# First-layer tiles in twos, with half-height fifth products side by side in the array

## Chip, cores and metric

The kernel runs on one core of one Trainium2 chip. The metric is the time on the device in microseconds, the median over runs. Profiles are single executions; times within one are counted from the start of its span.

## What is computed

```python
# attention part: a softmax over 7 taps per head, and a causal convolution with it
w = exp(weight_gen - max(weight_gen)) ; w = w / (sum(w) + 1e-9)      # (4, 4096, 8 heads, 7)
out[b, s, h, :] = sum_k w[b, s, h, k] * x_pad[b, s + k, h, :]         # 24 channels per head, 192 in all
# feed-forward part over 16384 tokens
h = x @ w_in                                                          # 192 -> 2048
g = where(h >= 1, h, where(h <= -1, 0, (h + 1)**2 / 4))
out = g @ w_out                                                       # 2048 -> 192
```

Both products are made from float32 values split into two parts, a high part in the type float32r and the rest (low), so that a product is high x high + low x high + high x low.

## The kernel before

**Tiling.** The 16384 tokens are taken in 32 groups of 512 tokens, and these in 16 pairs (b = 0, 1): the first and the last pair are written out, the others are a loop (over_pairs, L149). A group is four tokens on each of 128 partitions. The hidden width of 2048 is 16 tiles of 128 units (NT = 16).

**First layer.** The 192 input channels are 128 and a rest of 64. For each tile n, `hidden` (L570) makes five products of 128x128 weights by 128x512 columns into one PSUM bank (L581): main high x high, main low x high, main high x low, and two for the rest. The rest of 64 channels is stacked: the tile xt_rest holds the high parts on rows 0-63 and the low parts on rows 64-127, and in_rest_high and in_rest_low hold the same 64 rows of weights twice, on both halves. So the fourth product is high x high and high x low at once, and of the fifth (in_rest_low) only rows 0-63 (low x high) matter much.

**Gate.** ACT makes relu (L364) and its square (L370), DVE the gate in place in PSUM (L472), ACT the high part (L375, gate_high), DVE the low part (L478, gate_low). In a tile's step ACT does, in this order: relu of tile n, gate_high of tile n-1, in tile 2 the copies of the finished group's sums (take_cross, L390), square of tile n. DVE does gate_low of tile n-1, in tile 2 the sums (sum_outputs, L498), then the gate of tile n.

**Second layer.** `outputs` (L585, L601) makes, for tile n - 3 (LAG = 3), four times a product of 384 and one of 192 columns, into the four accumulator banks acc. In the last tile (15) of a group the 192-column product comes first. Tile 0 of a group waits, accumulator by accumulator, until DVE has summed the group before (out_summed).

**Banks.** Four PSUM banks (slot) are used in turn by tiles and transposes (uses, L167; slot_free, L200): each use waits until the use four back is finished, which for a tile is its gate_low and for a transpose the low part made by DVE (turned_rest, L482).

**Turns.** The next group's input is transposed on TensorE (turn, L557, L566) in two parts, behind the first layer of tiles 3 and 8 (TURN_AFTER); for the first two groups at other places (FIRST_TURNS_AFTER). ACT takes the high part (turned_top, L378, L382), DVE the low part (L487, L491). POOL makes the convolution that the turns read, a group or more ahead.

**Order on TensorE.** In each step: first layer of tile n, a turn if one is due, second layer of tile n - 3.

Of the kernel before, what the change touches and what calls it, by code (L numbers as in the profile page):

```python
# [13 lines left out]
F32 = mybir.dt.float32  # L14
F32R = mybir.dt.float32r
ALU = mybir.AluOpType
ACT = mybir.ActivationFunctionType
AX = mybir.AxisListType

P = 128  # L20
# [6 lines left out]
WARM_PRODUCTS, WARM_FROM = 10, 8  # L27
W_CHUNKS = 4
LAG = 3
TURN_AFTER = (3, 8)  # L30
FIRST_TURNS_AFTER = ((12, 14), (5, 10))
EVICT_AT = 2

SOFTMAX_AFTER = {3: (1,), 4: (2,), 6: (3, 4), 7: (5, 6)}
# [3 lines left out]
def build(nc, x, weight_gen, w_in, w_out, out):  # L38
# [7 lines left out]
    GT = TOK * P  # L46
# [3 lines left out]
    R = D - P  # L50
# [12 lines left out]
    with ExitStack() as ctx:  # L63
        def sb(name, shape, dt=F32):
            return ctx.enter_context(nc.sbuf_tensor(name, shape, dt))
# [19 lines left out]

        xt_high = [sb(f"xt_high{b}", [P, GT], F32R) for b in range(2)]
        xt_low = [sb(f"xt_low{b}", [P, GT], F32R) for b in range(2)]
        xt_rest = [sb(f"xt_rest{b}", [P, GT], F32R) for b in range(2)]

        in_main = sb("in_main", [P, FF])  # L90
# [4 lines left out]
        in_rest_high = sb("in_rest_high", [P, FF], F32R)  # L95
# [45 lines left out]
        def wait(eng, semaphore, pair, per_pair, offset):  # L141

            if isinstance(pair, int):
                if per_pair * pair + offset > 0:
                    eng.wait_ge(semaphore, per_pair * pair + offset)
            else:
                eng.wait_ge(semaphore, pair * per_pair + offset)
# [28 lines left out]
        def tile_slot(pair, b, n):  # L176
            return slot[(USES * b + uses(pair, b).index(("tile", n))) % SLOTS]

        def turn_slot(pair, b, part):

            if b == 0 and is_first(pair):
                return slot[2 + part]
            pair, b = before(pair, b)
            return slot[(USES * b + uses(pair, b).index(("turn", part))) % SLOTS]

        def before(pair, b):
            return (pair, 0) if b == 1 else (pair - 1, 1)
# [167 lines left out]
        @block.scalar  # L355
        def _(act):
            def exponent(pair, b):
                wait(act, softmax_step, pair, 2 * 5, 5 * b + 2)
                nc.scalar.activation(gen_exp[:], gen_shift[:], ACT.Exp).then_inc(exp_done, 1)

            def relu(pair, b, n):

                wait(act, hidden_done, pair, 2 * NT, NT * b + n + 1)
                nc.scalar.activation(half_relu[n % 2][:], tile_slot(pair, b, n)[:], ACT.Relu,  # L364
                                     scale=0.5, bias=0.5).then_inc(relu_done, 1)

            def squared(pair, b, n):
                wait(act, relu_done, pair, 2 * NT, NT * b + n + 1)
                wait(act, gate_done, pair, 2 * NT, NT * b + n - 1)
                nc.scalar.activation(square[n % 2][:], half_relu[n % 2][:], ACT.Square  # L370
                                     ).then_inc(square_done, 1)

            def gate_top(pair, b, n):
                wait(act, gate_done, pair, 2 * NT, NT * b + n + 1)
                nc.scalar.activation(gate_high[n % 4][:], tile_slot(pair, b, n)[:], ACT.Copy  # L375
                                     ).then_inc(gate_high_done, 1)

            def turned_top(pair, b, part):  # L378

                wait(act, turned, pair, 4, 2 * b + part + 1)  # L380
                dst = (xt_high, xt_rest)[part][b]
                nc.scalar.activation(dst[:], turn_slot(pair, b, part)[:], ACT.Copy  # L382
                                     ).then_inc(turned_high_done, 1)

            def take_cross(pair, b):

                for i in range(TOK):
                    wait(act, acc_done, pair, 2 * TOK, TOK * b + i + 1)
                    wait(act, out_summed, pair, 2 * TOK, TOK * (b - 1) + i + 1)
                    nc.scalar.activation(out_cross[:, i, :], acc[i][:, D:2 * D], ACT.Copy  # L390
                                         ).then_inc(cross_copied, 1)

            act.dma_start(gen_in[0][:].rearrange("p t k -> p (t k)"), w_runs[:, 0:TOK * HK]
                          ).then_inc(gen_loaded[0], 16)
            exponent(0, 0)

            for c in range(W_CHUNKS):
                cols = slice(c * CW, (c + 1) * CW)
                act.wait_ge(in_loaded[c], 48)
                for raw, high in ((in_main, in_main_high), (in_rest, in_rest_high)):  # L400
                    nc.scalar.activation(high[:, cols], raw[:, cols], ACT.Copy).then_inc(in_high_done, 1)

            def out_high(c):

                tiles = slice(c * CT, (c + 1) * CT)
                act.wait_ge(out_w_loaded[c], 16)
                nc.scalar.activation(out_parts[:, tiles, 0, :], out_raw[:, tiles, :], ACT.Copy
                                     ).then_inc(out_high_done, 1)

            out_high(0)  # L410
            out_high(1)
            turned_top(0, 0, 0)
            turned_top(0, 0, 1)
            exponent(0, 1)
            out_high(2)
            out_high(3)

            def body(pair):
                for b in range(2):
                    for n in range(NT):  # L420
                        relu(pair, b, n)
                        if n > 0:
                            gate_top(pair, b, n - 1)
                        elif not (b == 0 and is_first(pair)):
                            gate_top(*before(pair, b), NT - 1)
                        if n == EVICT_AT and not (b == 0 and is_first(pair)):
                            take_cross(*before(pair, b))
                        squared(pair, b, n)
                        if n == EXP_AFTER and not is_last(pair):
                            exponent(pair + 1, b)  # L430
                        if n in turn_after(pair, b):
                            turned_top(*after(pair, b), turn_after(pair, b).index(n))

            over_pairs(act, body)
            gate_top(PAIRS - 1, 1, NT - 1)
            take_cross(PAIRS - 1, 1)

        @block.vector
        def _(dve):
# [41 lines left out]

            def turned_rest(pair, b, part):  # L482

                wait(dve, turned_high_done, pair, 4, 2 * b + part + 1)
                src = turn_slot(pair, b, part)
                if part == 0:
                    nc.vector.tensor_tensor(xt_low[b][:], src[:], xt_high[b][:].bitcast(F32),  # L487
                                            ALU.subtract).then_inc(turned_low_done, 1)
                else:
                    low_rows = xt_rest[b][R:2 * R, :]  # L490
                    nc.vector.tensor_tensor(low_rows, src[R:2 * R, :], low_rows.bitcast(F32),  # L491
                                            ALU.subtract).then_inc(turned_low_done, 1)

            def sum_outputs(pair, b):
# [61 lines left out]
        def _(pe):  # L556
# [12 lines left out]

            def hidden(pair, b, n):  # L570

                slot_free(pe, pair, b, ("tile", n))
                if n == 0:
                    wait(pe, turned_low_done, pair, 4, 2 * b + 2)
                if b == 0 and is_first(pair) and n % CT == 0:
                    pe.wait_ge(in_low_done, 2 * (n // CT) + 2)
                units = slice(n * P, (n + 1) * P)
                products = ((in_main_high, xt_high), (in_main_low, xt_high), (in_main_high, xt_low),
                            (in_rest_high, xt_rest), (in_rest_low, xt_rest))
                for j, (w, xt) in enumerate(products):  # L580
                    ins = nc.tensor.matmul(tile_slot(pair, b, n)[:], w[:, units], xt[b][:],  # L581
                                           start=(j == 0), stop=(j == len(products) - 1))
                ins.then_inc(hidden_done, 1)

            def outputs(pair, b, n):  # L585

# [27 lines left out]
            def body(pair):  # L614
                for b in range(2):
                    for n in range(NT):
                        hidden(pair, b, n)
                        if n in turn_after(pair, b):
                            turn(*after(pair, b), turn_after(pair, b).index(n))
                        if n >= LAG:  # L620
                            outputs(pair, b, n - LAG)
                        elif not (b == 0 and is_first(pair)):
                            outputs(*before(pair, b), NT + n - LAG)

            over_pairs(pe, body)
            for n in range(NT - LAG, NT):
# [22 lines left out]
```

## Time and profile before

| | us |
|---|---|
| median of 3 runs | 1261.16 |
| lowest and highest run | 1260.84, 1261.38 |
| span of the profiled execution | 1259.3 |
| TensorE products busy in it | 1209.8 |
| ACT busy | 898.3 |
| DVE busy | 818.9 |
| POOL busy | 697.0 |

The span runs from the first to the last instruction of one execution. TensorE's products are pipelined: one starts before the end that is printed for the one before it, so the cost of a product in a string of them is the distance between two starts. PE is TensorE, PEld its weight loads, DVE VectorE, ACT ScalarE, POOL GpSimd. The granted clock of TensorE is 1.00 at 2.4 GHz.

### The profile page before, as it was taken

To read this page: it belongs to the slowest core of one execution; us is meant where nothing else is said; L and a number is where in the kernel's file an instruction comes from. 1 tells how busy PE (TensorE), PEld (TensorE's weight loads), DVE (VectorE), ACT (ScalarE), POOL (GpSimd) and SP (SyncE) were. 2 spreads that over 40 slices of the span, in tenths; PEclk is the share of its full clock that TensorE was granted. 3 is DMA by queue.
4 is the path that set the end of the run, shared out by engine and by line. 5 is a ranking of instruction groups with operands and counts; after the bars stand their busy time and mean duration, and the time that the engine had idled before them with its cause. 6 is when DMAs were issued, how large, how long until landed. Compare 5 with 4: busy or idle time off the path is not lost.

```text
span 1259.3 us, 21159 instructions
## 1 busy us (share of the span) xinstructions
PE 1209.8 (96%) x6932; PEld 1094.7 (87%) x6932; DVE 818.9 (65%) x1434; ACT 898.3 (71%) x1773; POOL 697.0 (55%) x450
## 2 busy tenths in 40 slices
PE   0699999999999999999999999999999999999998
PEld 0578999999999999999999999999999999999987
DVE  1886666666666666666666666666666666666565
ACT  0567777777777777777777777777777777777776
POOL 2496555775555775555776555676555676555500
PEclk9999999999999999999999999999999999999999
DMA  3311111001111101111101111101111100110000
GB/s 116 105 36 48 49 48 48 27 20 47 47 47 47 44 3 47 47 47 47 47 0 47 47 47 47 47 8 39 47 47 47 47 20 27 47 47 12 13 13 13
DMA packets 17426, 51.59 MB, mean 41 GB/s; under 512 B 1800, under 2 KB 8068, under 8 KB 17408
## 3 DMA queue, kind: packets, MB, share of 16 engines
q1 hardware_dynamic: 17264, 51.25, 11.9%
q8 instruction: 10, 0.16, 0.1%
q10 hardware_dynamic: 144, 0.11, 0.0%
q14 instruction: 8, 0.07, 0.0%
HBM read 38.77 MB, written 12.58 MB: 41 GB/s over the span
## 4 chain that ended last, share of the span: by engine, by line
PE 93%; SPq 3%; DVE 3%; DMA 1%; ACT 1%; issue 0%; DVEq 0%
PE slot L581 46%; PE acc L601 44%; PE slot L566 2%; SPq L240 1%; SPq L255 1%; DMA out_raw<-in_moe_w_out 1%; SPq L252 1%; DVE slot L472 1%; DVE gate_low L478 1%; DVE out_parts L515 0%; DVE in_main_low L508 0%; SPq L258 0%; DVE in_rest_low L508 0%; ACT gate_high L375 0%; SPq L223 0%
## 5 line engine op out<-in xcount | busy, mean ns | idle before, releaser
L601 PE MATMUL acc<-out_parts,gate_high 128*128 128x384 f32 x2048 | 616.4, 357 | 6.0 <-DVE gate_low L478 5.9
L478 DVE TENSOR_TENSOR gate_low<-slot,gate_high 128x512 fp32r<-128x512 f32 x512 | 353.7, 691 | 398.9 <-ACT gate_high L375 398.6
L601 PE MATMUL acc<-out_parts,gate_low 128*128 128x192 f32 x2048 | 513.7, 251 | 0.5 <-DVE gate_low L478 0.5
L364 ACT ACTIVATE half_relu<-slot 128x512 f32<-128x512 f32 x512 | 307.7, 601 | 288.5 <-PE slot L581 288.4
L601 PEld LDWEIGHTS acc<-out_parts,gate_high 128*128 128x128 f32 x2048 | 384.9, 188 | 27.1 <-DVE gate_low L478 8.4
L601 PEld LDWEIGHTS acc<-out_parts,gate_low 128*128 128x128 f32 x2048 | 390.3, 191 | 17.9 <-DVE gate_low L478 0.7
L472 DVE SCALAR_TENSOR_TENSOR slot<-slot,square 128x512 f32<-128x512 f32 x512 | 353.0, 690 | 3.9 <-ACT square L370 3.9
L370 ACT ACTIVATE square<-half_relu 128x512 f32<-128x512 f32 x512 | 325.2, 635 | 0.0
L375 ACT ACTIVATE gate_high<-slot 128x512 fp32r<-128x512 f32 x512 | 304.0, 594 | 25.6 <-DVE slot L472 25.4
L301 POOL TENSOR_TENSOR conv<-x_in,tap_w 128x768 f32<-128x768 f32 x31 | 47.8, 1542 | 482.3 <-DVE tap_w L462 468.4
L301 POOL TENSOR_TENSOR tap<-x_in,tap_w 128x768 f32<-128x768 f32 x186 | 289.6, 1564 | 0.0
L320 POOL TENSOR_TENSOR conv<-conv,tap 128x768 f32<-128x768 f32 x124 | 230.4, 1858 | 0.0
L581 PE MATMUL slot<-xt_high,in_main_high 128*128 128x512 f32 x512 | 211.7, 414 | 1.8 <-DVE xt_rest L491 1.5
L581 PE MATMUL slot<-xt_low,in_main_high 128*128 128x512 f32 x512 | 202.1, 395 | 0.0
L581 PE MATMUL slot<-xt_high,in_main_low 128*128 128x512 f32 x512 | 201.3, 393 | 0.0
L581 PE MATMUL slot<-xt_rest,in_rest_high 128*128 128x512 f32 x512 | 201.3, 393 | 0.0
L581 PE MATMUL slot<-xt_rest,in_rest_low 128*128 128x512 f32 x512 | 199.1, 389 | 0.0
L581 PEld LDWEIGHTS slot<-xt_rest,in_rest_low 128*128 128x128 f32 x512 | 96.2, 188 | 23.1
L581 PEld LDWEIGHTS slot<-xt_rest,in_rest_high 128*128 128x128 f32 x512 | 96.1, 188 | 22.3
L581 PEld LDWEIGHTS slot<-xt_low,in_main_high 128*128 128x128 f32 x512 | 96.3, 188 | 21.1
L581 PEld LDWEIGHTS slot<-xt_high,in_main_high 128*128 128x128 f32 x512 | 96.3, 188 | 2.6 <-DVE xt_rest L491 1.7
L581 PEld LDWEIGHTS slot<-xt_high,in_main_low 128*128 128x128 f32 x512 | 97.8, 191 | 0.1
(41 smaller groups left out, 493.4 us busy)
## 6 DMA issues: line engine op xcount, KB each, us to landing
x_in<-in_x SPq DMA_DIRECT2D x30, 960.0 KB
out<-out_sb SPq DMA_DIRECT2D x32, 384.0 KB, 2.6
gen_in<-in_weight_gen SPq DMA_DIRECT2D x31, 112.0 KB, 2.3
out_raw<-in_moe_w_out SPq DMA_DIRECT2D x4, 384.0 KB, 9.9
in_main<-in_moe_w_in SPq DMA_DIRECT2D x4, 256.0 KB, 4.7
in_rest<-in_moe_w_in SPq DMA_DIRECT2D x8, 128.0 KB, 7.6
x_in<-in_x SPq DMA_DIRECT2D x1, 768.0 KB
x_in<-in_x SPq DMA_DIRECT2D x4, 139.5 KB
```

The lines of the kernel that those rows point to most:

```text
L240: sp.dma_start(flat[lo + 1:lo + SEQ_PARTS, 0:before * D], x_runs[lo:lo + SEQ_PARTS - 1, (RUN - before) * D:RUN * D]).then_inc(x_loaded[b], 16)
L252: sp.dma_start(in_main[:, c * CW:(c + 1) * CW], w_in[0:P, c * CW:(c + 1) * CW]).then_inc(in_loaded[c], 16)
L301: ops.tensor_tensor(dst[:, :, 0:D].rearrange("p t (h c) -> p t h c", h=H), x_in[b][:, k:k + TOK, :].rearrange("p t (h c) -> p t h c", h=H) ...
L320: ops.tensor_tensor(to, conv[b][:, :, 0:D], tap[k % 3][:], ALU.add).then_inc(step_sem, 1)
L364: nc.scalar.activation(half_relu[n % 2][:], tile_slot(pair, b, n)[:], ACT.Relu, scale=0.5, bias=0.5).then_inc(relu_done, 1)
L370: nc.scalar.activation(square[n % 2][:], half_relu[n % 2][:], ACT.Square).then_inc(square_done, 1)
L375: nc.scalar.activation(gate_high[n % 4][:], tile_slot(pair, b, n)[:], ACT.Copy).then_inc(gate_high_done, 1)
L472: nc.vector.scalar_tensor_tensor(h[:], h[:], 1.0, square[n % 2][:], ALU.max, ALU.min).then_inc(gate_done, 1)
L478: nc.vector.tensor_tensor(gate_low[n % 4][:], tile_slot(pair, b, n)[:], gate_high[n % 4][:].bitcast(F32), ALU.subtract).then_inc(gate_low_ ...
L566: ins = nc.tensor.transpose(dst[:, i * P:(i + 1) * P], conv[b][:, i, part * P:(part + 1) * P], ident[:])
L581: ins = nc.tensor.matmul(tile_slot(pair, b, n)[:], w[:, units], xt[b][:], start=(j == 0), stop=(j == len(products) - 1))
L601: ins = nc.tensor.matmul(dst, stationary, moving, start=(n == 0 and j == 0), stop=(n == NT - 1 and j == 1))
```

## The change

Tiles are taken in twos, an even n and n + 1. `hidden` now makes four products for each tile. The fifth is moved into the new function `rest_lows`, which is called after the second layer in an even tile's step: it issues one product over rows 0-63 that ends the even tile's sum, and one over rows 64-127 that begins the odd tile's sum in its own PSUM bank. Then `hidden` of the odd tile adds four products to it, and the last one tells ACT that it is done. The high parts of the input's rest are needed on rows 64-127 too, so there is a tile xt_rest_top, and ACT copies the transposed rest in two halves of 64 rows instead of one of 128. The turns move to behind odd tiles.

```diff
-TURN_AFTER = (3, 8)
-FIRST_TURNS_AFTER = ((12, 14), (5, 10))
+TURN_AFTER = (3, 9)
+FIRST_TURNS_AFTER = ((11, 13), (5, 9))
...
+        xt_rest_top = [sb(f"xt_rest_top{b}", [P, GT], F32R) for b in range(2)]
...
-                dst = (xt_high, xt_rest)[part][b]
-                nc.scalar.activation(dst[:], turn_slot(pair, b, part)[:], ACT.Copy
-                                     ).then_inc(turned_high_done, 1)
+                src = turn_slot(pair, b, part)
+                if part == 0:
+                    nc.scalar.activation(xt_high[b][:], src[:], ACT.Copy).then_inc(turned_high_done, 1)
+                else:
+                    nc.scalar.activation(xt_rest_top[b][R:2 * R, :], src[R:2 * R, :], ACT.Copy
+                                         ).then_inc(turned_high_done, 1)
+                    nc.scalar.activation(xt_rest[b][0:R, :], src[0:R, :], ACT.Copy
+                                         ).then_inc(turned_high_done, 1)
...
-                wait(dve, turned_high_done, pair, 4, 2 * b + part + 1)
+                wait(dve, turned_high_done, pair, 6, 3 * b + 2 * part + 1)
...
-                    low_rows = xt_rest[b][R:2 * R, :]
-                    nc.vector.tensor_tensor(low_rows, src[R:2 * R, :], low_rows.bitcast(F32),
+                    nc.vector.tensor_tensor(xt_rest[b][R:2 * R, :], src[R:2 * R, :],
+                                            xt_rest_top[b][R:2 * R, :].bitcast(F32),
                                             ALU.subtract).then_inc(turned_low_done, 1)
...
-                slot_free(pe, pair, b, ("tile", n))
+                if n % 2 == 0:
+                    slot_free(pe, pair, b, ("tile", n))
...
-                            (in_rest_high, xt_rest), (in_rest_low, xt_rest))
+                            (in_rest_high, xt_rest))
                 for j, (w, xt) in enumerate(products):
+                    first, last = (j == 0, False) if n % 2 == 0 else (False, j == len(products) - 1)
                     ins = nc.tensor.matmul(tile_slot(pair, b, n)[:], w[:, units], xt[b][:],
-                                           start=(j == 0), stop=(j == len(products) - 1))
-                ins.then_inc(hidden_done, 1)
+                                           start=first, stop=last)
+                if n % 2:
+                    ins.then_inc(hidden_done, 1)
+
+            def rest_lows(pair, b, n):
+
+                slot_free(pe, pair, b, ("tile", n + 1))
+                if n == 0:
+                    wait(pe, turned_high_done, pair, 6, 3 * b + 3)
+                nc.tensor.matmul(tile_slot(pair, b, n)[:], in_rest_low[0:R, n * P:(n + 1) * P],
+                                 xt_rest[b][0:R, :], start=False, stop=True).then_inc(hidden_done, 1)
+                nc.tensor.matmul(tile_slot(pair, b, n + 1)[:],
+                                 in_rest_low[R:2 * R, (n + 1) * P:(n + 2) * P],
+                                 xt_rest_top[b][R:2 * R, :], start=True, stop=False)
...
                             outputs(*before(pair, b), NT + n - LAG)
+                        if n % 2 == 0:
+                            rest_lows(pair, b, n)
```

## Rows read from the trace of the kernel before

**Rows 1.** The page, part 1: busy time, share of the span, instructions.
```profile
PE 1209.8 (96%) x6932; PEld 1094.7 (87%) x6932; DVE 818.9 (65%) x1434; ACT 898.3 (71%) x1773; POOL 697.0 (55%) x450
```
**Rows 2.** The page, part 4: the chain that ended last, by line.
```profile
PE slot L581 46%; PE acc L601 44%; PE slot L566 2%; SPq L240 1%; SPq L255 1%; DMA out_raw<-in_moe_w_out 1%; SPq L252 1%; DVE slot L472 1%; DVE gate_low L478 1%; DVE out_parts L515 0%; DVE in_main_low L508 0%; SPq L258 0%; DVE in_rest_low L508 0%; ACT gate_high L375 0%; SPq L223 0%
```
**Rows 3.** Stretches, one of a pair of groups: window, its us, busy us, clock.
```profile
671.00:746.00 75.00, 75.00 (x433) 68.03 (x433) 49.41 (x88) 55.47 (x111) 44.25 (x28) 1.00 0.12 40
```
**Rows 4.** Timeline of TensorE: start, duration, line, out<-in; two tiles.
```profile
640.61 0.41 PE L581 MATMUL slot<-xt_high,in_main_high 128*128 128x512 f32 x1
...
641.55 0.39 PE L581 MATMUL slot<-xt_rest,in_rest_low 128*128 128x512 f32 x1
641.78 0.33 PE L601 MATMUL acc<-out_parts,gate_high 128*128 128x384 f32 x1
...
642.81 0.25 PE L601 MATMUL acc<-out_parts,gate_low 128*128 128x192 f32 x1
642.89 0.41 PE L581 MATMUL slot<-xt_high,in_main_high 128*128 128x512 f32 x1
643.15 0.39 PE L581 MATMUL slot<-xt_high,in_main_low 128*128 128x512 f32 x1
...
645.19 0.41 PE L581 MATMUL slot<-xt_high,in_main_high 128*128 128x512 f32 x1
```
**Rows 5.** Timeline of TensorE's weight loads, same place.
```profile
642.81 0.19 PEld L581 LDWEIGHTS slot<-xt_high,in_main_high 128*128 128x128 f32 x1
642.92 0.19 PEld L581 LDWEIGHTS slot<-xt_high,in_main_low 128*128 128x128 f32 x1
```
**Rows 6.** Timeline of TensorE, first group: products behind an idle stretch.
```profile
67.20 0.47 PE L581 MATMUL slot<-xt_high,in_main_high 128*128 128x512 f32 x1 [0.34 <-DVE in_rest_low L508]
67.50 0.40 PE L581 MATMUL slot<-xt_high,in_main_low 128*128 128x512 f32 x1
```
**Rows 7.** Timeline of TensorE, start of a group: tiles 2 and 3.
```profile
620.29 0.25 PE L601 MATMUL acc<-out_parts,gate_low 128*128 128x192 f32 x1
...
622.61 0.60 PE L566 MATMUL slot<-ident,conv 128*128 128x128 f32 x4
622.97 0.42 PE L601 MATMUL acc<-out_parts,gate_high 128*128 128x384 f32 x1
```
**Rows 8.** Timeline of ACT: tile 2 of that group, and a later tile.
```profile
620.49 0.60 ACT L364 ACTIVATE half_relu<-slot 128x512 f32<-128x512 f32 x1 [0.69 <-PE slot L581]
620.98 0.59 ACT L375 ACTIVATE gate_high<-slot 128x512 fp32r<-128x512 f32 x1
621.46 1.01 ACT L390 ACTIVATE out_cross<-acc 128x192 f32<-128x192 f32 x4
...
641.98 0.60 ACT L364 ACTIVATE half_relu<-slot 128x512 f32<-128x512 f32 x1 [0.68 <-PE slot L581]
```
**Rows 9.** Timeline of DVE: tile 2 of that group.
```profile
621.61 0.69 DVE L478 TENSOR_TENSOR gate_low<-slot,gate_high 128x512 fp32r<-128x512 f32 x1 [0.99 <-ACT gate_high L375]
622.22 1.14 DVE L498 TENSOR_TENSOR out_sb<-acc,out_cross 128x192 f32<-128x192 f32 x4
```
**Rows 10.** Waits of the whole span: who waited for whom, us, times, longest.
```profile
PE acc L601 <- DVE gate_low L478: 6.4, 4, 3.7
```
**Rows 11.** Groups by line, 600 to 1000 us: the turned rest, the main part.
```profile
L491 DVE TENSOR_TENSOR xt_rest<-slot,xt_rest 64x512 fp32r<-64x512 f32 x11 | 7.6, 695 | 0.3
L487 DVE TENSOR_TENSOR xt_low<-slot,xt_high 128x512 fp32r<-128x512 f32 x10 | 6.8, 680 | 0.0
L382 ACT ACTIVATE xt_rest<-slot 128x512 fp32r<-128x512 f32 x10 | 6.0, 600 | 0.0
```
**Rows 12.** Timeline at the end: the last tile's second layer.
```profile
1254.36 0.36 PE L601 MATMUL acc<-out_parts,gate_low 128*128 128x192 f32 x1 [0.47 <-DVE gate_low L478]
```

## Prediction

> **What bounds the kernel now.** I read the page's busy times first: TensorE's products fill 1209.8 us of a span of 1259.3 us [rows 1]. The chain that ended last says the same by line: the first layer's products (L581) are 46% of the span, the second layer's (L601) 44% [rows 2]. The stretches settle it: from 671 to 746 us, which is one pair of groups, TensorE is busy 75.00 of 75.00 us at a granted clock of 1.00 [rows 3]. So the steady part is a string of matmuls, and the only price that counts is the distance from one start to the next. The durations printed (0.39 us and so on) overlap, so I never sum them.
>
> From the timeline of TensorE [rows 4]: a tile starts its first layer at 640.61 and the next at 642.89, 2.28 us; two tiles take 4.58 us. The fifth product starts at 641.55 and the second layer at 641.78, so that product costs 0.23 us. Two tiles' fifth products are 0.46 us: all that this change can touch on TensorE. A 192-column product costs 0.08 (642.81 to 642.89), the second layer of a tile 1.11, and four first-layer products 0.94.
>
> **The pair of half-height products.** There are 32 groups of 16 tiles, so 256 pairs. Call c what the two 64-row products cost together, from the first one's start to the start of the next tile's first product. The pairs give 256 x (c - 0.46) us. The trace has no product on 64 rows, so c has to be bounded.
> - Lower end: both stream at once and nothing is lost: one product, 0.23.
> - The second one needs its own weight load. Loads stand 0.11 us apart where they are closest (642.81 and 642.92) [rows 5], and a product starts 0.08 to 0.17 after its load. That puts the second product some 0.09 to 0.17 behind the first: c = 0.32 to 0.40.
> - No overlap at all: 0.46. The number of loads does not fall (26 in a pair, before and after).
> - If TensorE must empty itself on going from 128 rows to 64 and again on going back: a 192-column product ends, as modelled, 0.25 us after its start against 0.08 to the next start, and a 512-column one 0.39 against 0.23 [rows 4], so each crossing adds about 0.16: c = 0.23 + 0.32 = 0.55. A start from empty adds more: the tile at 67.20, which follows an idle stretch, has 0.30 to its second product, where 0.26 is usual [rows 6]. With that and the staggered second load c reaches about 0.8.
>
> I take c = 0.46. It is the middle of 0.23 and 0.68, and the nearest row in kind is the fifth product itself. It stands for a second product 0.17 behind the first and 0.06 lost at the borders, and equally for two products that don't overlap.
>
> The row for a change of kind speaks mildly for a cheap border: four transposes between first and second layer take 0.36 us (622.61 to 622.97), 0.09 each, hardly more than products of that width would, so there is no large gap at that change of mode [rows 7]. The Trainium skill speaks against the edit here: "TensorEngine Tiling (Array Packing)", section Key Properties, says that a change of tiling mode, as against a change of tile, makes TensorE drain. No row of this trace shows such a change; with that rule the time would be that of the second rival below.
>
> **What the new order does to the end of a group.** This is the part a busy share hides. Before, an even tile's first layer ended ahead of the second layer of three tiles back; now its last product comes behind it. Look at tile 2 of a group, where ACT also fetches the finished group's sums (L390). The second layer of the old group's tile 15 starts at 620.29 (known by its 192-column product coming first), and tile 2's relu on ACT at 620.49 [rows 7, 8]. ACT is in order: behind that relu stand gate_high of tile 1 (620.98) and then the four copies of the sums (from 621.46). DVE then does gate_low of tile 1 at 621.61 and the sums (L498) from 622.22, 1.73 us after the relu [rows 8, 9]. The first sum is done about 0.35 + 0.05 later, 2.13 after the relu (622.62), and the new group's first second-layer product, which overwrites that accumulator, starts at 622.97 [rows 7]. So the present slack is 0.35 us.
>
> Now tile 2's last product starts only after the 1.16 us of tile 15's second layer; call that start r. The relu comes 0.39 + 0.04 behind (as 641.55 to 641.98 does), so the first sum is ready at r + 0.43 + 2.13 = r + 2.56. TensorE is there at r + c + 0.94 + 0.36 (tile 3's four products, the transposes) = r + 1.30 + c. It waits 1.25 - c us: 1.02 at c = 0.23, 0.79 at 0.46. Everything on TensorE queues behind it. It happens in groups 1 to 31: 31 x (1.25 - c). The other sums follow each other faster (about 0.26) than TensorE asks for them (0.29), so only the first one counts.
>
> **Other places.** Today TensorE waits for gate_low 4 times, 6.4 us in all, at the two ends of the run [rows 10].
> - The slots: behind a transpose a tile takes the slot of three tiles back. Tile 6 needs gate_low of tile 3, which stands on ACT behind tile 4's relu: 0.43 + 0.49 + 0.63 + 0.69 + 0.05 = 2.29 us after tile 4's half-height product, and TensorE arrives c + 0.94 + 1.11 = 2.05 + c after it. Nothing for c of 0.24 or more; the same for tile 12. The wait of the pair for the odd tile's slot sits behind a second layer that needs the same gate_low or an earlier stall: nothing.
> - One more copy on ACT per group (0.60 us, 64 rows costing what 128 do by L491 against L487, 695 and 680 ns) [rows 11]: it lies behind tile 9's square, and ACT idles 0.68 us before each relu there, some 2 us over the next tiles [rows 8]. DVE's subtraction waits only for the first half. Nothing. In the opening it delays the exponent and the weights' split by up to 0.5 us, hidden or not.
> - The turns at 9 instead of 8 and the first ones at 11 and 13: the convolution they read is done long before. Nothing.
> - The last tile: its chain through ACT now starts behind tile 14's. TensorE waited before tile 15's second layer until 1254.36, 0.47 us [rows 12]; some 0.5 to 1 us more. I take 1.
>
> **Sum.** The span is 1259.3 us and the median of the runs 1261.16, 1.9 us more; I add the change to the median. Time = 1261.2 + 256 (c - 0.46) + 31 (1.25 - c) + 1 = 1183.2 + 225 c. At c = 0.46: 1286.7. Even where the pair is perfect the wait at the group's start takes back 32 us of 59. The kernel gains only if c is under 0.35.
>
> **Rivals.**
> - It gains: the two products really run side by side, c = 0.23 to 0.33. For it: loads are taken ahead of running products in this trace [rows 5], and there is no visible gap at the transposes. Against it: the loads are spaced 0.11, and both borders must be free. It decides at c = 0.35. 1235 to 1257, at best 1234.9. The skill's "TensorE: Matmul & The Clock Gate", Part 3, says tiles at different rows start some 4 ns apart; that would be this rival's best end, and no run so far shows it.
> - TensorE empties at both borders: c = 0.55 to 0.82, the time 1307 to 1368, at 0.68 1336. For it: two crossings per pair are 512 chances to lose 0.16. Against it: the transposes.
> - The pair costs as forecast, but the wait at the group's start is not there (ACT or DVE has more room than I read): 1261.2 + 256 x 0 + 1 = 1262, no change. Against it: ACT's order is fixed in the program, and its rows carry the 1.73 us.
> - That the edit does not do what it says, two half-height products one after the other, is inside the forecast (c = 0.46).
>
> **Chances.** Forecast, c from 0.34 to 0.54 (1260 to 1305, likeliest 1286.7): 0.37. Gain: 0.28. Emptying: 0.28. No wait at the start of a group: 0.07. The range leaves out the best tip of the first rival and the upper half of the second: 1237 to 1337. A difference under 0.2% (2.5 us) could not be told from none; for that strip around c = 0.35 and the third rival I give 0.09. Faster 0.28, slower 0.63.
>
> **What would show it.** In the changed profile: (1) the distance from the first half-height product to the next tile's first one is c; (2) the distance between the starts of the two tells overlap from stagger; (3) a distance over 0.09 from the last 192-column product to the first half-height one is a border loss; (4) TensorE idles 0.8 us before the first second-layer product of each group behind DVE L498, 31 times; (5) the granted clock stays 1.00; (6) a pair of tiles takes 4.12 us + c. I am wrong if c is under 0.34 or over 0.54, or if (4) is missing or larger than 1.3 us.

## The result, and the profile after

| | us |
|---|---|
| before, median | 1261.0 |
| after, median of 4 runs | 1334.47 (1332.88 to 1335.25) |
| ratio after to before | 1.0581 (95% interval 1.0566 to 1.0596) |
| span of the profiled execution, after | 1331.1 |

The change costs 73.5 us. The direction was forecast and the size was not: 1286.7 had been predicted, 26 us over the kernel before. The time lies just inside the upper end of the range, in the second rival's field.

The page of the kernel after, part 1 (busy time, share, instructions) and one line of part 4 (the chain that ended last, by line):

```profile
PE 1261.5 (95%) x6932; PEld 1050.6 (79%) x6932; DVE 820.2 (62%) x1434; ACT 922.1 (69%) x1805; POOL 696.4 (52%) x450
...
PE acc L621 43%; PE slot L589 36%; PE slot L599 8%; ACT gate_high L376 2%; PE slot L572 1%; DVE out_sb L504 1%; SPq L241 1%; SPq L256 1%; DMA out_raw<-in_moe_w_out 1%; SPq L253 1%; DVE gate_low L484 1%; ACTq L148 0%; DVE slot L478 0%; DVEq L148 0%; SPq L259 0%
```

In the kernel after, L589 is the first layer, L599 and L601 are the two half-height products, L621 is the second layer and L572 the transposes; on ACT, L365 is the relu, L376 gate_high and L396 the copies of the sums; on DVE, L484 is gate_low and L504 the sums.

TensorE still has most of the chain that ended last, with as many products as before ([rows 1], x6932) and 52 us more of busy time. Two things are new: the half-height products have 8% of the chain by themselves (L599), and gate_high on ACT (L376, 2%) and the sums on DVE (L504, 1%) stand in it; before, gate_high had under 1% and the sums nothing [rows 2].

A stretch of TensorE's timeline in the kernel after (start, duration, line, output<-inputs), the end of an even tile's step and the odd tile's first layer. It answers to [rows 4]:

```profile
644.46 0.25 PE L621 MATMUL acc<-out_parts,gate_low 128*128 128x192 f32 x1
644.63 0.50 PE L599 MATMUL slot<-xt_rest,in_rest_low 64*128 64x512 f32 x1
644.64 0.50 PE L601 MATMUL slot<-xt_rest_top,in_rest_low 64*128 64x512 f32 x1
645.07 0.50 PE L589 MATMUL slot<-xt_high,in_main_high 128*128 128x512 f32 x1
645.40 0.40 PE L589 MATMUL slot<-xt_high,in_main_low 128*128 128x512 f32 x1
...
649.37 0.50 PE L599 MATMUL slot<-xt_rest,in_rest_low 64*128 64x512 f32 x1
```

The two half-height products start together (644.63, 644.64). So the change does what it says. But the first one starts 0.17 us after the 192-column product (0.08 is usual), the next 128-row product 0.43 after them (0.23 is usual), and the one behind that 0.33 after (0.23). A border is a place where the string goes from products on 128 rows to products on 64, or back. At the two borders 0.09 + 0.20 + 0.10 = 0.39 us are lost, against 0.23 saved. From pair to pair it is 4.74 us, where it was 4.58 [rows 4].

The weight loads in the same place show what goes with it. A bracket is idle time ahead of a load, and "issue" means that no semaphore held it:

```profile
644.63 0.18 PEld L599 LDWEIGHTS slot<-xt_rest,in_rest_low 64*128 64x128 f32 x1 [0.16 <-issue]
644.64 0.18 PEld L601 LDWEIGHTS slot<-xt_rest_top,in_rest_low 64*128 64x128 f32 x1
645.06 0.19 PEld L589 LDWEIGHTS slot<-xt_high,in_main_high 128*128 128x128 f32 x1 [0.24 <-issue]
645.17 0.19 PEld L589 LDWEIGHTS slot<-xt_high,in_main_low 128*128 128x128 f32 x1
```

In the rest of the string a load is taken ahead, while the product before it runs (642.92 for the product at 643.15, rows 4 and 5 of before). At a border the load starts with its own product: it was not taken ahead. The two half-height loads start together, on different rows.

The other new cost is at the start of a group, where the timeline of TensorE, ACT and DVE together (kernel after) answers to [rows 7] to [rows 9]:

```profile
693.87 0.50 PE L599 MATMUL slot<-xt_rest,in_rest_low 64*128 64x512 f32 x1
...
694.40 0.60 ACT L365 ACTIVATE half_relu<-slot 128x512 f32<-128x512 f32 x1 [1.20 <-PE slot L599]
...
694.90 0.60 ACT L376 ACTIVATE gate_high<-slot 128x512 fp32r<-128x512 f32 x1
...
695.33 0.60 PE L572 MATMUL slot<-ident,conv 128*128 128x128 f32 x4
695.38 1.01 ACT L396 ACTIVATE out_cross<-acc 128x192 f32<-128x192 f32 x4
...
696.13 1.14 DVE L504 TENSOR_TENSOR out_sb<-acc,out_cross 128x192 f32<-128x192 f32 x4
...
696.54 0.44 PE L621 MATMUL acc<-out_parts,gate_high 128*128 128x384 f32 x1 [0.60 <-DVE out_sb L504]
```

From tile 2's relu (694.40) to the first sum on DVE (696.13) it is 1.73 us, as in the kernel before. TensorE has issued its transposes at 695.33; they take 0.36, so it could have gone on at 695.69 and goes on at 696.54: 0.85 us. The waits of the whole span (who waited for whom, us, times, longest) have it 31 times, in every group but the first; their microseconds are counted from the modelled end of a product, so they are shorter than the 0.85 by starts:

```profile
PEld acc L621 <- DVE out_sb L504: 23.2, 28, 0.8
PE acc L621 <- DVE out_sb L504: 19.5, 31, 1.1
DVE xt_rest L496 <- ACT xt_rest L388: 14.7, 32, 0.5
```

The last line is a small miss of mine and shows no cost on the path: DVE's subtraction waits for both copies of the turned rest, not for the first alone, and idles 0.46 us a group.

### The profile page after: what moved, and what is told of

Its sections match the earlier page's. It is cut to its first block, busy times and chain, and to the rows that moved or that the text cites. A ratio compares the mean times of both kernels' runs of the same rounds, so it can differ in the third digit from the quotient of the medians.

```text
span 1331.1 us, 21222 instructions
## 1 busy us (share of the span) xinstructions
PE 1261.5 (95%) x6932; PEld 1050.6 (79%) x6932; DVE 820.2 (62%) x1434; ACT 922.1 (69%) x1805; POOL 696.4 (52%) x450
## 4 chain that ended last, share of the span: by engine, by line
PE 89%; SPq 3%; DVE 3%; issue 2%; ACT 2%; DMA 1%; ACTq 0%; DVEq 0%
PE acc L621 43%; PE slot L589 36%; PE slot L599 8%; ACT gate_high L376 2%; PE slot L572 1%; DVE out_sb L504 1%; SPq L241 1%; SPq L256 1%; DMA out_raw<-in_moe_w_out 1%; SPq L253 1%; DVE gate_low L484 1%; ACTq L148 0%; DVE slot L478 0%; DVEq L148 0%; SPq L259 0%
## 5 line engine op out<-in xcount | busy, mean ns | idle before, releaser
L621 PE MATMUL acc<-out_parts,gate_high 128*128 128x384 f32 x2048 | 617.8, 357 | 23.8 <-DVE out_sb L504 19.5
L484 DVE TENSOR_TENSOR gate_low<-slot,gate_high 128x512 fp32r<-128x512 f32 x512 | 353.7, 691 | 455.7 <-ACT gate_high L376 455.7
L621 PE MATMUL acc<-out_parts,gate_low 128*128 128x192 f32 x2048 | 513.7, 251 | 0.6 <-DVE gate_low L484 0.6
L365 ACT ACTIVATE half_relu<-slot 128x512 f32<-128x512 f32 x512 | 308.1, 602 | 259.4 <-PE slot L599 259.4
L621 PEld LDWEIGHTS acc<-out_parts,gate_high 128*128 128x128 f32 x2048 | 384.9, 188 | 53.2 <-DVE out_sb L504 23.2
L621 PEld LDWEIGHTS acc<-out_parts,gate_low 128*128 128x128 f32 x2048 | 390.4, 191 | 20.0 <-DVE gate_low L484 0.8
L376 ACT ACTIVATE gate_high<-slot 128x512 fp32r<-128x512 f32 x512 | 304.8, 595 | 102.5 <-DVE slot L478 102.5
L589 PE MATMUL slot<-xt_high,in_main_high 128*128 128x512 f32 x512 | 235.9, 461 | 2.6 <-DVE xt_rest L496 2.2
L589 PE MATMUL slot<-xt_high,in_main_low 128*128 128x512 f32 x512 | 203.7, 398 | 0.0
L589 PE MATMUL slot<-xt_low,in_main_high 128*128 128x512 f32 x512 | 202.6, 396 | 0.0
L589 PE MATMUL slot<-xt_rest,in_rest_high 128*128 128x512 f32 x512 | 201.9, 394 | 0.0
L589 PEld LDWEIGHTS slot<-xt_high,in_main_high 128*128 128x128 f32 x512 | 96.0, 187 | 66.0 <-issue 63.5
L601 PE MATMUL slot<-xt_rest_top,in_rest_low 64*128 64x512 f32 x256 | 127.6, 498 | 0.0
L599 PE MATMUL slot<-xt_rest,in_rest_low 64*128 64x512 f32 x256 | 126.7, 495 | 0.0
L589 PEld LDWEIGHTS slot<-xt_rest,in_rest_high 128*128 128x128 f32 x512 | 96.5, 189 | 23.9
L589 PEld LDWEIGHTS slot<-xt_low,in_main_high 128*128 128x128 f32 x512 | 96.6, 189 | 23.0
L589 PEld LDWEIGHTS slot<-xt_high,in_main_low 128*128 128x128 f32 x512 | 97.6, 191 | 0.1
```

The lines of the kernel that those rows point to most:

```text
L484: nc.vector.tensor_tensor(gate_low[n % 4][:], tile_slot(pair, b, n)[:], gate_high[n % 4][:].bitcast(F32), ALU.subtract).then_inc(gate_low_ ...
L599: nc.tensor.matmul(tile_slot(pair, b, n)[:], in_rest_low[0:R, n * P:(n + 1) * P], xt_rest[b][0:R, :], start=False, stop=True).then_inc(hid ...
L601: nc.tensor.matmul(tile_slot(pair, b, n + 1)[:], in_rest_low[R:2 * R, (n + 1) * P:(n + 2) * P], xt_rest_top[b][R:2 * R, :], start=True, st ...
L621: ins = nc.tensor.matmul(dst, stationary, moving, start=(n == 0 and j == 0), stop=(n == NT - 1 and j == 1))
```

## The experiments

Theory A: the loss is two separate prices, the borders between 128-row and 64-row products (some 0.18 us per pair beyond what the overlap saves) and the wait at the start of 31 groups. Rivals: the new order alone, or half-height products slow in themselves, or never side by side.

**The new order without half-height products.** Both products of `rest_lows` over all rows:

```diff
-                nc.tensor.matmul(tile_slot(pair, b, n)[:], in_rest_low[0:R, n * P:(n + 1) * P],
-                                 xt_rest[b][0:R, :], start=False, stop=True).then_inc(hidden_done, 1)
+                nc.tensor.matmul(tile_slot(pair, b, n)[:], in_rest_low[:, n * P:(n + 1) * P],
+                                 xt_rest[b][:], start=False, stop=True).then_inc(hidden_done, 1)
...
-                                 in_rest_low[R:2 * R, (n + 1) * P:(n + 2) * P],
-                                 xt_rest_top[b][R:2 * R, :], start=True, stop=False)
+                                 in_rest_low[:, (n + 1) * P:(n + 2) * P],
+                                 xt_rest[b][:], start=True, stop=False)
```

> The changed kernel's order, but both products of rest_lows run over all 128 rows, as the fifth product did before. Same sums as in the kernel before, no 64-row product anywhere. Theory A (two parts: the borders between 128-row and 64-row products cost 0.175 us per pair net of the overlap, 45 us in all, and the wait at the start of a group costs about 0.85 us, 31 times, 26 us): the borders go, the wait stays or grows by 0.05, so 1261 + 31 x 0.9 + 1, about 1290. Rival B (the loss is made by the new order alone, in waits on ACT and DVE, and the half-height products cost no more than one product): 1334 or more, since this kernel has one product more per pair.

Measured: 1290.67 us, ratio 1.0231 (1.0214 to 1.0248). Its two fifth products run one after the other, so TensorE has the time of one product more per pair, and it is 43.8 us faster than the changed kernel. The same place in this kernel, TensorE's timeline, and its waits:

```profile
645.85 0.25 PE L621 MATMUL acc<-out_parts,gate_low 128*128 128x192 f32 x1
645.94 0.41 PE L599 MATMUL slot<-xt_rest,in_rest_low 128*128 128x512 f32 x1
646.20 0.39 PE L601 MATMUL slot<-xt_rest,in_rest_low 128*128 128x512 f32 x1
646.42 0.40 PE L589 MATMUL slot<-xt_high,in_main_high 128*128 128x512 f32 x1
646.66 0.40 PE L589 MATMUL slot<-xt_high,in_main_low 128*128 128x512 f32 x1
```
```profile
PE acc L621 <- DVE out_sb L504: 18.9, 31, 1.1
```

No border, and the 31 waits are all there. The rival that the order alone makes the loss is out. The start of a group here, TensorE, ACT and DVE together:

```profile
673.87 0.39 PE L599 MATMUL slot<-xt_rest,in_rest_low 128*128 128x512 f32 x1
...
674.30 0.60 ACT L365 ACTIVATE half_relu<-slot 128x512 f32<-128x512 f32 x1 [1.02 <-PE slot L599]
...
675.26 0.60 PE L572 MATMUL slot<-ident,conv 128*128 128x128 f32 x4
676.03 1.14 DVE L504 TENSOR_TENSOR out_sb<-acc,out_cross 128x192 f32<-128x192 f32 x4
...
676.43 0.44 PE L621 MATMUL acc<-out_parts,gate_high 128*128 128x384 f32 x1 [0.57 <-DVE out_sb L504]
```

The relu comes 0.43 behind the even tile's fifth product, and TensorE waits from 675.62 (675.26 + 0.36) to 676.43: 0.81 us.

**The sums fetched first.** The changed kernel with ACT's copies and DVE's sums moved to the front of tile 2's step:

```diff
+                        if n == EVICT_AT and not (b == 0 and is_first(pair)):
+                            take_cross(*before(pair, b))
                         relu(pair, b, n)
                         if n > 0:
                             gate_top(pair, b, n - 1)
                         elif not (b == 0 and is_first(pair)):
                             gate_top(*before(pair, b), NT - 1)
-                        if n == EVICT_AT and not (b == 0 and is_first(pair)):
-                            take_cross(*before(pair, b))
...
+                        if n == EVICT_AT and not (b == 0 and is_first(pair)):
+                            sum_outputs(*before(pair, b))
                         if n > 0:
                             gate_rest(pair, b, n - 1)
```

> The changed kernel, with ACT's four copies of the finished group's sums put ahead of tile 2's relu, and DVE's sums ahead of gate_low of tile 1. Theory A: the first sum is ready before the pair of tile 2 is over, the 31 waits behind L504 vanish, about 26 us less than the changed kernel: 1308. Rival B (the wait only moves: the pair of tile 4 then waits for gate_low of tile 2): over 1325, and a new wait of about 0.8 us a little later in each group.

Measured: 1306.39 us, ratio 1.0356 (1.0339 to 1.0373). 28.1 us less than the changed kernel, 0.91 per group, and no wait of TensorE behind L504 is left in the trace. The wait did not move elsewhere; that rival, over 1325, is out.

**Both edits.**

> Both edits at once: the changed kernel's order with products over 128 rows, and the sums fetched ahead of tile 2's relu. If the borders and the wait at the group's start are all there is, this is back at the kernel before: 1261 to 1263. A rest of over 5 us would be a third cost of the new order.

Measured: 1259.28 us, ratio 0.9988 (0.9978 to 0.9998). There is no third cost. The four kernels make a square: the borders cost 43.8 us with the wait and 47.1 without it (0.17 and 0.18 per pair), the wait 28.1 us with the borders and 31.4 without (0.91 and 1.01 per group). The 1.01 is not all wait. By the traces a steady pair takes 4.58 us in the kernel with the new order alone (643.89 to 648.47) and 4.56 in this one (644.08 to 648.64), and 0.02 in each of 8 pairs is 0.16 us of a group.

**The pair of products ahead of the second layer.** The changed kernel with the call of `rest_lows` moved up by one step:

```diff
+                        if n % 2 == 0:
+                            rest_lows(pair, b, n)
                         if n >= LAG:
                             outputs(pair, b, n - LAG)
                         elif not (b == 0 and is_first(pair)):
                             outputs(*before(pair, b), NT + n - LAG)
-                        if n % 2 == 0:
-                            rest_lows(pair, b, n)
```

> The changed kernel, with rest_lows called ahead of the second layer instead of behind it, so a pair of half-height products stands between a 512-column product and a 384-column one. Theory A: tile 2's relu comes 1.1 us earlier against TensorE, so the wait at the group's start vanishes, the borders stay: about 1308, and a pair of tiles takes 4.75 us as in the changed kernel. Rival B (what is lost at a border depends on the neighbours, the short 192-column product in front hides part of it): over 1320.

Measured: 1311.05 us, ratio 1.0393 (1.0376 to 1.041), under the 1320 from which the border would have depended on its neighbours. Also in this way the wait at the group's start is gone and the borders stay, in other company: a 512-column product in front, the second layer behind. Two lines of its waits, and the border in its timeline:

```profile
PEld slot L599 <- DVE gate_low L484: 55.6, 128, 2.2
...
PE slot L599 <- DVE gate_low L484: 7.0, 29, 1.7
```
```profile
643.80 0.39 PE L589 MATMUL slot<-xt_rest,in_rest_high 128*128 128x512 f32 x1
644.12 0.50 PE L599 MATMUL slot<-xt_rest,in_rest_low 64*128 64x512 f32 x1
644.12 0.50 PE L601 MATMUL slot<-xt_rest_top,in_rest_low 64*128 64x512 f32 x1
644.55 0.36 PE L621 MATMUL acc<-out_parts,gate_low 128*128 128x192 f32 x1
```

The border costs about the same: 0.32 from the 512-column product (0.09 over 0.23), then 0.43 again. It is 4.7 us slower than the kernel with the sums fetched first; here the pair, one second layer earlier, waits for the odd tile's bank 29 times, 7.0 us in all. Of the 3 us over the 1308 expected that is the likely cause; it was not tried apart and is not shown.

**The lower half alone.** The kernel before, in its old order, with the fifth product on rows 0-63 and nothing beside it:

```diff
                 for j, (w, xt) in enumerate(products):
-                    ins = nc.tensor.matmul(tile_slot(pair, b, n)[:], w[:, units], xt[b][:],
+                    rows = slice(0, R if j == 4 else P)
+                    ins = nc.tensor.matmul(tile_slot(pair, b, n)[:], w[rows, units], xt[b][rows, :],
```

> The kernel before, in its old order, with the fifth product of each tile over rows 0-63 alone (the product of the two low parts is left out). Theory A (any change of the number of rows is a border, for the lower half of the array too): 512 border pairs of 0.4 us each, about 1261 + 205 = 1466. Rival B (rows 0-63 are a 128-row product with part of the rows idle, only rows 64-127 change the array): 1261.

Measured: 1453.91 us, ratio 1.1528 (1.1509 to 1.1547). Half the rows in one product of each tile, and 193 us more: 192.8 / 512 = 0.377 us for a stretch of one half-height product, between two borders, over the 128-row product that it replaces. Expected were 0.40. TensorE's timeline:

```profile
640.47 0.39 PE L582 MATMUL slot<-xt_rest,in_rest_high 128*128 128x512 f32 x1
640.79 0.50 PE L582 MATMUL slot<-xt_rest,in_rest_low 64*128 64x512 f32 x1
641.22 0.44 PE L602 MATMUL acc<-out_parts,gate_high 128*128 128x384 f32 x1
641.50 0.25 PE L602 MATMUL acc<-out_parts,gate_low 128*128 128x192 f32 x1
```

The distances are those of the pair: 0.32, 0.43, 0.28. So the price is not that of the upper rows or of two banks at once. What is left is the going from 128 rows to 64 and back, or half-height products that are slow in themselves; the next run parts these two.

**Two pairs in one stretch.** The changed kernel with the pair issued twice in a row, so the low x high part of the rest is in the sum twice:

```diff
+                for again in range(2):
+                    (rows 0-63 into the bank of tile n)
+                    (rows 64-127 into the bank of tile n + 1)
```

> The changed kernel with the pair of half-height products issued twice in a row (the low x high part of the rest is added twice). Theory A (the cost sits in the borders, and inside the 64-row stretch two products side by side take the time of one): 256 x 0.23 more, less 31 x 0.23 of shorter waits: 1334 + 52 = 1386. Rival B (half-height products are slow in themselves, 0.43 us for each pair): 1334 + 256 x 0.43 - 31 x 0.43, about 1431.

Measured: 1386.71 us, ratio 1.0994 (1.0976 to 1.1013).

```profile
644.06 0.50 PE L600 MATMUL slot<-xt_rest,in_rest_low 64*128 64x512 f32 x1
644.06 0.50 PE L604 MATMUL slot<-xt_rest_top,in_rest_low 64*128 64x512 f32 x1
644.40 0.39 PE L600 MATMUL slot<-xt_rest,in_rest_low 64*128 64x512 f32 x1
644.40 0.39 PE L604 MATMUL slot<-xt_rest_top,in_rest_low 64*128 64x512 f32 x1
644.73 0.50 PE L589 MATMUL slot<-xt_high,in_main_high 128*128 128x512 f32 x1
```

The stretch is 0.67 us instead of 0.43, so the second pair costs 0.24: two products for the time of one. The borders are paid once per stretch, and half-height products are not slow in themselves. The step from pair to pair grows by a little less, from 4.75 to 4.96 (medians over the two traces).

That the total came out at the 1386 expected is luck, though. I had 256 x 0.23 for the pairs, less 31 x 0.23 for shorter waits at the groups' starts. The waits did not get shorter; this kernel's line (L624 is its second layer), beside 19.5 us in the changed kernel:

```profile
PE acc L624 <- DVE out_sb L504: 19.7, 31, 1.1
```

Here the even tile is only done with the second round, so its relu comes later by as much as TensorE does. 256 x 0.21 = 54 us and nothing off is what the trace gives, for 52.2 measured: one term was too large and the other should not have been there.

**Both on the same rows.** Half-height products that can't lie side by side:

```diff
-                                 in_rest_low[R:2 * R, (n + 1) * P:(n + 2) * P],
-                                 xt_rest_top[b][R:2 * R, :], start=True, stop=False)
+                                 in_rest_low[0:R, (n + 1) * P:(n + 2) * P],
+                                 xt_rest[b][0:R, :], start=True, stop=False)
```

> The changed kernel with both half-height products on rows 0-63. Theory A (the two really run at the same time when they are on different rows, and one after the other on the same rows): 256 x 0.23 more, less 31 x 0.23: about 1386, their starts 0.23 apart. Rival B (they were never side by side, the equal start times are only the record): 1334, no change.

Measured: 1380.51 us, ratio 1.0949 (1.0931 to 1.0968); 46 us over the changed kernel, where 52 were expected. TensorE's timeline, then its loads:

```profile
640.70 0.49 PE L599 MATMUL slot<-xt_rest,in_rest_low 64*128 64x512 f32 x1
641.04 0.39 PE L601 MATMUL slot<-xt_rest,in_rest_low 64*128 64x512 f32 x1
641.36 0.50 PE L589 MATMUL slot<-xt_high,in_main_high 128*128 128x512 f32 x1
```
```profile
640.70 0.18 PEld L599 LDWEIGHTS slot<-xt_rest,in_rest_low 64*128 64x128 f32 x1 [0.16 <-issue]
640.81 0.19 PEld L601 LDWEIGHTS slot<-xt_rest,in_rest_low 64*128 64x128 f32 x1
```

On the same rows the products start 0.34 apart and the loads 0.11; on different rows both pairs start together. The overlap in the changed kernel is real. And within the stretch the load is taken ahead again (640.81 for the product at 641.04).

The 6 us between 46 and 52 are in the pairs. The waits are shorter, as expected, by 6.8 us (19.5 in the changed kernel):

```profile
PE acc L621 <- DVE out_sb L504: 12.7, 31, 0.9
```

But a pair takes 4.96 us here against 4.75 (medians over the two traces), 0.21 more and not 0.23: 256 x 0.21 - 6.8 = 47 us.

**Every second pair.** The kernel with the sums fetched first, half-height products in the pairs of tiles 0, 4, 8 and 12 only, 128-row products in the others.

> The changed kernel's order with the sums fetched ahead of tile 2's relu; every second pair (tiles 0, 4, 8 and 12) uses two half-height products, the others two over 128 rows. Theory A (a fixed price per stretch of half-height products, 0.18 us net of the overlap, from the difference of two runs, 1306.4 - 1259.3 over 256): 1259.3 + 128 x 0.184 = 1282.8. Rival (a cost that depends on how long ago the array was last changed, or on the clock): a number away from the middle, over 1290 or under 1275.

Measured: 1285.35 us, ratio 1.0188 (1.0173 to 1.0204): (1285.35 - 1259.28) / 128 = 0.20 us per stretch, against 0.18 with all of them. A price per stretch, nearly the same when there are half as many. A pair with 128-row products in this kernel's trace:

```profile
641.16 0.41 PE L589 MATMUL slot<-xt_high,in_main_high 128*128 128x512 f32 x1
...
645.74 0.41 PE L589 MATMUL slot<-xt_high,in_main_high 128*128 128x512 f32 x1
```

It takes 4.58 us, 0.02 more than the 4.56 in the kernel with both edits, and 128 x 0.02 = 2.6 us is what the total lies over the sum. So the excess is in the pairs without a border; why these take 4.58 stays open.

**Where the small gain of both edits is from.** The kernel before, with its products untouched and the sums fetched first, and beside it the kernel with both edits once more:

> The kernel before, its products untouched, with the sums fetched ahead of tile 2's relu (ACT) and ahead of gate_low of tile 1 (DVE). If the fetching order gave the small gain of the run with both edits: about 1259. If that gain is from the order of products in twos: 1261, or more, since ACT now holds tile 2's relu back until the second layer of tile 15 is done.

> The kernel with 128-row products in the new order and the sums fetched first, once more, beside the run above. The order in twos puts two fifth products and four first-layer products in one row of six, so one product per pair loses its place behind a 192-column one: 1259 again, 0.1 to 0.2% under the kernel before.

Measured: 1260.59 us, ratio 0.9995 (0.9986 to 1.0004), for the first, 1258.86 us, ratio 0.9984 (0.9975 to 0.9993), for the second. Fetching first gives nothing measurable in the old order; with the order in twos as well, the kernel is 2.4 us (0.2%) under the kernel before, at the limit of what can be told from no change. Its pair takes 4.56 us, in both its traces, where it was 4.58 [rows 4]; over 256 pairs 0.01 to 0.02 us is about that much. The order alone doesn't show it: in the one trace without the fetching first the pair took 4.58. My reason for it, one product per pair that no longer follows a 192-column one, does not hold in its timeline: two products per pair still have the 0.26 us distance, as before. What the gain is from stays open.

## Why the prediction was right or wrong

**The bound: right.** TensorE's starts set the time. The traces give 4.74 - 4.56 = 0.18 us for a pair and 0.85 for a wait, so 256 x 0.18 + 31 x 0.85 = 46 + 26 = 72 us between the kernel with both edits and the changed one. The runs have 1334.47 - 1259.28 = 75.2.

**The pair's price c: the step that failed.** The forecast took c = 0.46, with "0.06 lost at the borders", and 0.39 us were lost there. The runs give, beside two full-height products at 0.46, 0.17 to 0.18 more: c = 0.64 in the sense of the sum. That is 256 x 0.18 = 46 us that the forecast lacked. The stagger that I had put into the same c was not there, and that hid part of the miss from my own first sign: the distance from the first half-height product to the next tile's first one is 0.43, inside the 0.34 to 0.54 that I had called right. It holds only one of the three losses, because the entry (0.09) lies ahead of it and the late second product (0.10) behind it. The third sign (0.17 where 0.09 was the limit) and the sixth (4.74 = 4.12 + 0.62) show them.

The price I had put on emptying, 0.55 with 0.16 per crossing, and 0.04 for a start from empty (0.30 against 0.26, [rows 6]), adds up to 0.59, not far from 0.64, but its parts are others: 0.09 on the way in, 0.20 on the way out, 0.10 behind. The reason I gave for a cheap border was the wrong row: transposes between products [rows 7] are a change of kind, but they use all 128 rows, and they show nothing about a change of rows. The nearest row was that of a start from empty [rows 6], which I used only for the upper end: 0.30 to the second product there, 0.33 behind the border here.

What TensorE does at a border, as far as the runs show it: the next weight load is not taken ahead, and the first product after it has 0.50 us in the record instead of 0.39. The Trainium skill, "TensorEngine Tiling (Array Packing)", section Key Properties, says that a change of tiling mode makes TensorE drain. The trace agrees with that rule, with 0.09 and 0.20 us lost at the two borders, and by the 0.377 us of the run with the lower half alone, a half-height product on rows 0-63 with nothing beside it counts as a change too. How much of the 0.39 us is the emptying and how much the weight load that is not taken ahead, the records, whose ends are modelled, do not say.

**The side-by-side part: right in mechanism, and I had staggered it wrongly.** I expected the second product 0.09 to 0.17 behind the first, since loads stand 0.11 apart [rows 5]. That spacing is for loads on the same rows; on different rows both loads and both products start together. The Trainium skill's "TensorE: Matmul & The Clock Gate", Part 3, says some 4 ns between such tiles. The records show 0 to 10 ns: here the trace agrees.

**The wait at the start of a group: right in mechanism, place and count; its size was right without borders and short with them.** 31 waits behind L504, as said, and from relu to first sum 1.73 us, as said. The formula, 1.25 - c (2.56 - 1.30 is 1.26, a slip of 0.01 us), gives 0.79 at c = 0.46, and the kernel with the new order alone, where c is 0.46, waits 0.81. With the borders it gives 0.61 at c = 0.64, and 0.85 was measured. Two terms were missing, both read off the rows at 693.87 to 696.54. The relu comes 0.53 behind the half-height product and not 0.43, as a product behind a border is recorded longer: 0.10. And the price of entering the stretch lies ahead of r, the first half-height product, so it gives DVE no time: TensorE is done with the transposes at r + 1.82 (695.69), not at r + 1.94: 0.12. With the 0.61 they make 0.83. By the runs' medians it is 0.91 a group; the 2 us between 31 x 0.85 and 28.1 are within the spread of the changed kernel's runs (1332.88 to 1335.25). Against the formula at c = 0.64 the sum lacked 31 x 0.24, some 7 us.

**The rivals.** Gain: out, and c under 0.35 was never near. Emptying: a price at both borders is what happened. That 1336 stood beside it, with c = 0.68, is near 1334.5 by luck: at c = 0.64 my formula says 1327, and the wait, forecast too short by those 7 us, makes up the rest. That the time lies inside the stated range is no credit either, since the case that I held likeliest, 1260 to 1305, did not come. I gave emptying 0.28 because two mechanisms pulled to the middle and I took the middle as a case of its own, which it was not: the price of a border is either there or not. No wait at the group's start: out.

**Costs put at nothing.** The slots: no wait behind them in the changed kernel's timeline of the steady part; they show as soon as the pair is moved up (29 waits, 7.0 us). The extra ACT copy: no wait of TensorE in the list of waits comes from it. The clock: a mean of 0.997 granted, 0.998 in the profile before, so all this is at 2.4 GHz.

## What to carry to other kernels

A short stretch of half-height products between full-height ones costs its two borders, here about 0.39 us, and each pair in it saves 0.23: one pair per stretch loses, and two would about break even (0.39 + 2 x 0.23 = 0.85 against 0.92; an estimate from these rows, as the run with two pairs adds one and replaces nothing). So such products pay only where they can be gathered. When a bound for an unknown cost has two mechanisms behind it, take the price of one or of the other, not the middle. And when a tile's last product moves behind other work, look up what stands in order behind that tile's first reader: here four copies on ACT that had nothing to do with the tile, worth 28 us, and cheap to move (in the old order, where nobody waited for them, moving them gave nothing).

## What the hardware showed that I had not expected

- A 512-column product on 64 rows in each tile instead of one on 128 made the kernel 15% slower: 0.377 us for each.
- Two weight loads on different halves of the rows start together (644.06 and 644.06 in the kernel with two pairs), where the closest loads on the same rows stand 0.11 us apart.
- A product behind a border is recorded with 0.50 us, and the one behind it starts 0.33 to 0.34 later. Behind an idle stretch it was 0.47 us and 0.30 [rows 6].
